# Reading y twice out of its PSUM bank instead of once through a copy in SBUF

## The reference, cut to what matters

```python
x = softmax(q @ agents.T) @ (softmax(agents @ k.T) @ v)      # attention, scaled
h = x @ w_in1
g = where(h >= 1, h, where(h <= -1, 0, (h + 1) ** 2 / 4))
y = g @ w_out1                                                # end of the first layer
r = maximum(y @ w_in2, 0)
out = (s * r * r + b) @ w_out2
```

## Time and profile before

| | |
|---|---|
| time, median of 3 executions | 1171.68 us (1171.39 to 1171.7) |
| the profiled execution's own time | 1169.62 us |
| its span | 1167.8 us |
| PE busy | 1146.8 us, 98% of the span |
| ACT, DVE, POOL busy | 927.0, 914.8 and 822.5 us |
| mean granted clock of PE | 0.955 of full |

### The profile page before, as it was taken

The page is one execution under the profiler, slowest core; times in us unless marked ns, Lnnn a source line. Parts: engine busy times, 40 slices in busy tenths (PEclk is TensorE's granted clock), DMA queues, the critical chain, the costliest instruction groups (busy, mean ns, idle before and its releaser), DMA issues.

```text
span 1167.8 us, 18729 instructions
## 1 busy us (share of the span) xinstructions
PE 1146.8 (98%) x5188; PEld 958.1 (82%) x5188; DVE 914.8 (78%) x1461; ACT 927.0 (79%) x1748; POOL 822.5 (70%) x1214
## 2 busy tenths in 40 slices
PE   9997899999999999999999999999999999999998
PEld 9996678888878888788878887888888887888886
DVE  2433788888878888888878887888788888888876
ACT  1213888888888888888888888888888888888887
POOL 0160078788778788778878887887787887888770
PEclk6556999999999999999999999999999999999999
DMA  9510000000000000000000000000000000000000
GB/s 369 188 63 1 1 1 18 1 19 18 19 2 18 18 0 18 18 0 18 18 18 1 18 18 1 18 18 0 18 18 18 0 18 19 0 18 9 4 6 19
DMA packets 12275, 30.48 MB, mean 26 GB/s; under 512 B 1616, under 2 KB 8240, under 8 KB 11824
## 3 DMA queue, kind: packets, MB, share of 16 engines
q1 hardware_dynamic: 12208, 29.81, 7.5%
HBM read 23.40 MB, written 6.40 MB: 26 GB/s over the span
## 4 chain that ended last, share of the span: by engine, by line
PE 88%; ACT 5%; issue 4%; DVE 3%; DMA 0%; ACTq 0%; SPq 0%; DVEq 0%
PE ps_h L471 7%; PE ps_h L473 7%; PE ps_h L472 7%; PE ps_y L434 7%; PE ps_o L504 7%; PE ps_o L502 7%; PE ps_o L503 7%; PE ps_h L452 7%; PE ps_h L453 7%; PE ps_y L436 7%; PE ps_y L435 7%; PE ps_y L371 4%; PE ps_h L355 3%; PE ps_job L334 1%; ACT sb_g_hi L571 1%
## 5 line engine op out<-in xcount | busy, mean ns | idle before, releaser
L836 POOL TENSOR_TENSOR sb_g_lo<-sb_square,sb_g_hi 128x500 fp32r<-128x500 f32 x380 | 484.2, 1274 | 31.7
L717 DVE SCALAR_TENSOR_TENSOR ps_h<-sb_square,ps_h 128x500 f32<-128x500 f32 x400 | 272.3, 681 | 119.3 <-ACT sb_square L551 116.8
L571 ACT ACTIVATE sb_g_hi<-ps_h 128x500 fp32r<-128x500 f32 x400 | 235.7, 589 | 124.0 <-DVE ps_h L717 109.2
L699 DVE SCALAR_TENSOR_TENSOR sb_g_lo<-ps_h,sb_g_hi 128x500 fp32r<-128x500 f32 x400 | 271.0, 678 | 34.7 <-ACT sb_g_hi L571 25.5
L704 DVE TENSOR_SCALAR sb_below<-ps_h 128x500 f32<-128x500 f32 x384 | 259.4, 676 | 10.4 <-PE ps_h L453 9.5
L576 ACT ACTIVATE sb_relu<-ps_h 128x500 f32<-128x500 f32 x400 | 235.5, 589 | 19.6 <-PE ps_h L473 9.6
L551 ACT ACTIVATE sb_square<-sb_below 128x500 f32<-128x500 f32 x400 | 247.3, 618 | 0.8 <-DVE sb_below L704 0.3
L585 ACT ACTIVATE sb_square<-sb_relu 128x500 f32<-128x500 f32 x400 | 246.7, 617 | 0.6
L834 POOL TENSOR_SCALAR sb_g_hi<-sb_square 128x500 fp32r<-128x500 f32 x380 | 228.2, 600 | 0.0
L833 POOL TENSOR_TENSOR sb_gate<-sb_ones 1x1 f32<-1x1 f32 x380 | 70.1, 185 | 181.1 <-ACT sb_square L585 179.5
L434 PE MATMUL ps_y<-sb_g_hi,sb_w_out_hi 128*128 128x500 f32 x400 | 161.9, 405 | 5.0 <-DVE sb_y L739 2.6
(11 more groups left out here) (85 smaller groups left out, 1339.9 us busy)
## 6 DMA issues: line engine op xcount, KB each, us to landing
sb_q_ring<-in_q SPq DMA_DIRECT2D x25, 250.0 KB, 2.8
out<-sb_out_ring SPq DMA_DIRECT2D x25, 250.0 KB, 2.1
sb_kv_ring<-in_k SPq DMA_DIRECT2D x12, 512.0 KB, 8.2
sb_kv_ring<-in_v SPq DMA_DIRECT2D x12, 512.0 KB, 7.5
sb_w_in<-in_moe_w_in SPq DMA_DIRECT2D x1, 1024.0 KB, 15.6
sb_w_stage<-in_moe_w_out SPq DMA_DIRECT2D x4, 256.0 KB, 5.7
sb_w_stage<-in_moe_w_in SPq DMA_DIRECT2D x1, 1024.0 KB, 7.8
sb_w_stage<-in_moe_w_out SPq DMA_DIRECT2D x1, 1024.0 KB, 4.8
```

The lines of the kernel that those rows point to most:

```text
L571: nc.scalar.activation(g1_hi[:, place % SPLIT_RING], h1_ps[place % H1_BANKS][:, 0:W], ACT.Relu).then_inc(g1_hi_ready, 1)
L699: nc.vector.scalar_tensor_tensor(g1_lo[:, place % SPLIT_RING], h1_ps[place % H1_BANKS][:, 0:W], 0.0, as_f32(g1_hi[:, place % SPLIT_RING]), ...
L717: nc.vector.scalar_tensor_tensor(h, square1[:, place % WORK_RING], 1.0, h, ALU.min, ALU.add).then_inc(g1_summed, 1)
L836: nc.gpsimd.tensor_tensor(g2_lo[:, place % SPLIT_RING], square, as_f32(hi), ALU.subtract).then_inc(g2_split, 1)
```

## The change

The copy L739 and the tile `y_sb` go. ACT rounds `y` to `y_hi` straight out of the bank, at the end of step j = 1 in every iteration, and waits for the last matmul into the bank. DVE subtracts out of the bank as well, at the end of step j = 1, where the copy stood, and waits for `y_hi`. PE's L434 at j = 2 waits for the subtraction (`y_split`) instead of the copy.

```diff
-        y_sb = sb("y", [128, W])
...
-        y_ready = sem("y_ready")
...
-        def one_mlp(i):
-            return isinstance(i, int) and (i == 1 or i >= CHUNKS)
...
                     if f == 0:

-                        at_least(pe, y_ready, i)
+                        at_least(pe, y_split, i)
...
-                    if j == (LAG1 - 1 if one_mlp(i) else LAG1) and chunk(i, phase, -1)[2]:
-                        act.wait_ge(y_ready, i)
-                        nc.scalar.copy(y_hi[:, (phase - 1) % CHUNKS_PER_TRIP], y_sb[:]).then_inc(y_hi_ready, 1)
+                    if j == LAG1 - 1 and chunk(i, phase, -1)[2]:
+                        act.wait_ge(g1_used, i * TILES)
+                        nc.scalar.copy(y_hi[:, (phase - 1) % CHUNKS_PER_TRIP], y_ps[:, 0:W]).then_inc(y_hi_ready, 1)
...
                     if j == LAG1 - 1 and chunk(i, phase, -1)[2]:
-                        dve.wait_ge(g1_used, i * TILES)
-                        if not isinstance(i, int) or i >= 2:
-                            dve.wait_ge(y_split, i - 1)
-                        nc.vector.tensor_copy(y_sb[:], y_ps[:, 0:W]).then_inc(y_ready, 1)
-                    if j == (LAG1 if one_mlp(i) else LAG1 + 1) and chunk(i, phase, -1)[2]:
                         slot = (phase - 1) % CHUNKS_PER_TRIP
                         dve.wait_ge(y_hi_ready, i)
-                        nc.vector.tensor_tensor(y_lo[:, slot], y_sb[:], as_f32(y_hi[:, slot]), ALU.subtract).then_inc(y_split, 1)
+                        nc.vector.tensor_tensor(y_lo[:, slot], y_ps[:, 0:W], as_f32(y_hi[:, slot]), ALU.subtract).then_inc(y_split, 1)
```

## The result

The changed kernel takes 1188.54 us in the median of 4 executions (1187.24 to 1189.61), the kernel before 1171.54 (1169.37 to 1171.7, 4 executions). The ratio is 1.0149 with a 95% interval of 1.0131 to 1.0167: 17.0 us slower by the medians, 15.3 to 19.6 by the interval. The profiled execution has a span of 1185.4 us against 1167.8, 17.6 more. One execution of the kernel before, among those beside the experiments, took 2795 us where its others took 1166 to 1172, and no ratio uses it.

What follows compares the result with a forecast made beforehand. PE's matmuls bound the steady part, so only PE's standing still counts. Plain iterations 12.8, first iterations of a trip 8.4, less 2.7 coming back, plus 0.15 in iteration 1: 18.6 us, giving 1190.3; range 1183 to 1200.

Steps and rivals of the forecast that it cites:

- The rounding on ACT: On ACT, `y_hi` starts 0.52 us after L585 starts, 0.84 us after the bank is complete, and takes 0.63 us.
- The subtraction: On DVE, it starts at 556.39 and takes 0.67 us, as L699 does, within bounds of 0.67 and 1.18 us.
- PE in plain iterations: In 15 plain iterations L434 comes 0.66 us later, 0.76 us with its weight load; 0.68 us in iterations 2 and 24.
- The first iterations of a trip: In six first iterations of a loop trip, L434 comes at 600.27 instead of 598.87: 6 x 1.40 = 8.4 us.
- What comes back: At L471, the second layer's first matmul, the wait for L743 goes in seven places: 7 x 0.39 = 2.7 us.
- The ring: L717 of step 2 on DVE starts 1.47 us late; PE does not wait, and it is caught up by step 4.
- The rival that ACT's place decides: On ACT, a rounding starting before 555.10, 0.13 us before L585, costs nothing in a plain iteration; some 1168 us, 6%.
- The rule on the bank: The single bank for `y` stalls PE for its whole emptying: 24 x (2.14 - 0.68) = 35 us, 1207.
- (b): On DVE, POOL holds the subtraction to 1.18 us like L743: 12 us more, 1202; 8%.
- (c): DVE's 1.47 us lateness is not caught up, so a second L434 or L471 waits each iteration: 12 us more, about 1202; 8%.
- (a): ACT rounds when the bank is complete instead of behind L585, so L434 does not wait: some 1168 us; 6%.
- (d): The stall at L434 is smaller: 14.7 us, 1186, or 1180 if PE regained half of it later; 8%.

## Why the prediction was right

The forecast was 18.6 us more than before. The span grew by 17.6, the median by 17.0, and 1188.5 us was measured where 1190.3 was forecast. By its own steps:

- **What bounds the kernel**: right. DVE's saved 21.8 us of busy time are worth nothing in the loop, which the run with the work put back shows as well (0.3 us over 21 iterations).
- **The rounding on ACT**: it starts 0.51 us behind the second square (0.52 forecast). It took 0.57 us against bounds of 0.57 to 0.61, and from start to start it is 0.60 us to the subtraction, not 0.63. This is most of what was off, 0.03 in each of 24 places, 0.7 us.
- **The subtraction**: 0.68 us beside a working POOL, as L699 in the earlier trace rows and not as L743 in the earlier trace rows. The rival with 1.18 us falls. The spare subtraction with both operands in SBUF at step 3 took 1.27 us in its median beside a working POOL, and 0.67 in iteration 1, where POOL does nothing. So the difference takes two things together: both operands in SBUF, and POOL at work. The Trainium skill, SBUF — State Buffer, section SBUF: two separate sides, which the prediction weighed, says that a DVE operation with two SBUF inputs and a GpSimd operation that reads SBUF shut each other out for a whole instruction. The traces agree with it in 1.27 against 0.67 and 0.68.
- **PE in plain iterations**: 0.71 us measured against 0.76; iterations 2 and 24 cost 0.64 against 0.68. The first iterations of a trip: 1.69 - 0.30 = 1.39 of idle time against 1.40; from start to start it is 1.38 in the mean of the six. PE took up its matmul 0.13 us after the subtraction's end, as forecast. The sum of these is 15 x 0.71 + 2 x 0.64 + 6 x 1.38 = 20.2 against 21.2.
- **What comes back**: the wait of the second layer is gone everywhere, 2.7 us, and the run with the copy and an earlier subtraction loses it too, 3.0 us with an interval of 1.5 to 4.6, 2.4 from the first matmul. With it the sum is 17.5, and iteration 1 is 0.1 longer: 17.6 us, which is what the span grew by. That it meets to 0.1 us is luck, since other steps differ by some tenths of a us both ways, among them a stall of 0.4 us near the end that the kernel before did not have at that place.
- **The ring**: it was late by 1.4 us (1.47 forecast), and PE did not wait for it. The run with the subtraction behind the sum takes the larger part of that lateness away and gains 0.6 us.
- **The rival that ACT's place decides**: the prediction said that a rounding started 0.13 us or more ahead of the second square costs nothing in a plain iteration. (By its own times it is 0.14: 555.24 against 555.10.) The three runs with the rounding moved bear the mechanism out: with one square ahead of it a plain iteration still loses 0.21 us, with none ahead nothing.
- **The rule on the bank**: a stall of the whole emptying would have been 35 us, and the span grew by 17.6. PE's 1.61 us of other matmuls cover most of the emptying, and only what sticks out was paid, 0.71 us in a plain iteration. The Trainium skill, Perfetto Trace Analysis, section Matmuls under Optimizing Tensor Performance, advises to rotate groups of matmuls through banks; no run here has a second bank for `y`.
- **The range**: it ends at 1200, and the rivals (b) and (c) were both priced at about 1202, so it left out the whole of them and not just their upper ends. With (a) and the lower half of (d) that is up to 26 in 100 left out, not 2 in 10.

What the prediction did not have is the clock. With the waits 0.6 us longer, as in the run with the subtraction twice, a forecast by lengths was too low by about 3 us of 17.5. That the waits of the changed kernel stayed short of this was not foreseen.

## What to carry to other kernels

When an operation is dropped between a bank and the matmul that wants it back, write down when each remaining reader can start on its own engine, in program order: the removed copy was cheap because DVE was free the moment the bank was complete, and its replacement had to wait behind two squares on ACT. Move such a reader forward in its engine's order before giving up the idea; here the same instructions with the rounding ahead of the relu are 0.3% faster than the kernel with the copy. Look for a second wait that the edit removes in passing, since it may be had alone. And before reading a difference of a few us out of medians of four executions, lay the profiles side by side from a common point in the program: here that turned 8.7 us into 5.1.

## What the runs showed of the hardware

A stall of the tensor engine of about 2.2 us can be followed by about 3.4 us at a granted clock of 0.50 (1.2 GHz), which cost 1.5 us more. Behind equal waits of 2.2 us in one execution it happened in 9 of 17 iterations, behind 3.4 us in all six, three of which had 6.8 us at 0.50 and lost 2.4 to 3.2 us; behind 1.69 us, in the changed kernel's profile, the six first iterations of a trip took 43.4 to 43.6 us with no such step. What decides between equal waits stays open.

A higher mean clock did not mean a shorter time: of the changed kernel's four executions those with a mean granted clock of 0.957 took 1187.2 and 1187.5 us, those with 0.996 and 0.997 took 1189.6. In the profiles the difference lies ahead of the loop: the first matmul L447 stands at 100.6 us in the changed kernel (clock 0.50 in most of the start) and at 103.5 with the subtraction behind the sum (1.00 throughout). The other profiles fall in line: the four whose clock was 1.00 all through the start have it at 103.3 to 103.6 us, the seven others, at 0.50 for part or most of it, at 98.1 to 101.1. Why the start is longer at the higher clock was not tried.
